# First-layer activation of a two-layer kernel: the square of r moves to ScalarE, and VectorE's two passes become one

## Time and profile before

| what | value |
|---|---|
| median of 3 runs | 1155.81 us (1155.42 to 1156.33) |
| the profiled execution's own time | 1150.71 us |
| span of the profiled execution | 1149.0 us |
| mean granted TensorE clock over the span | 0.993 of full speed |
| busy: TensorE / VectorE / ScalarE | 1125.8 / 947.9 / 630.8 us |
| HBM traffic over the span | 13.70 MB read, 6.29 MB written |

### The profile page before, as it was taken

The page is one execution under the profiler, slowest core; times in us unless marked ns, Lnnn a source line. Parts: engine busy times, 40 slices in busy tenths (PEclk is TensorE's granted clock), DMA queues, the critical chain, the costliest instruction groups (busy, mean ns, idle before and its releaser), DMA issues.

```text
span 1149.0 us, 23218 instructions
## 1 busy us (share of the span) xinstructions
PE 1125.8 (98%) x9746; PEld 951.0 (83%) x9746; DVE 947.9 (83%) x858; ACT 630.8 (55%) x627; POOL 3.4 (0%) x16
## 2 busy tenths in 40 slices
PE   5999999999999999999999999999999999999998
PEld 3777878888888888888888888888888888888886
DVE  7998998978888798888888798887888878866665
ACT  4545655555565655555555555555555555565544
POOL 1000000000000000000000000000000000000000
PEclk8998999999999999999999999999999999999999
DMA  6002300100001000000000000000000000000000
GB/s 183 1 1 65 93 1 1 29 29 1 1 1 29 28 1 1 1 29 28 1 2 1 29 29 1 1 1 29 29 1 2 1 29 1 1 1 1 29 1 28
DMA packets 12423, 21.33 MB, mean 19 GB/s; under 512 B 1073, under 2 KB 5169, under 8 KB 12337
## 3 DMA queue, kind: packets, MB, share of 16 engines
q1 hardware_dynamic: 12256, 19.99, 6.1%
q0 software_dynamic: 64, 0.00, 0.0%
q10 hardware_dynamic: 16, 0.00, 0.0%
HBM read 13.70 MB, written 6.29 MB: 17 GB/s over the span
## 4 chain that ended last, share of the span: by engine, by line
PE 88%; DVE 8%; issue 3%; ACT 1%; DMA 0%; SPq 0%; DVEq 0%; ACTq 0%
PE acc L717 28%; PE h L670 23%; PE h L683 18%; PE acc_rem L732 18%; DVE g L445 3%; DVE g L453 1%; DVE mixed L502 1%; DMA xraw_rem<-in_x 0%; ACT g_hi L303 0%; DVE mixed_rem L516 0%; DVE mixed L516 0%; DVE up_lo L551 0%; DVE up_rem_lo L551 0%; DVE g_lo L463 0%; DVE dn_lo L551 0%
## 5 line engine op out<-in xcount | busy, mean ns | idle before, releaser
L303 ACT ACTIVATE g_hi<-g 128x1024 fp32r<-128x1024 f32 x128 | 135.8, 1061 | 218.8 <-DVE g L453 218.7
L447 DVE SCALAR_TENSOR_TENSOR g<-r,scale,h 128x1024 f32<-128x1024 f32 x128 | 161.9, 1278 | 69.5 <-ACT r L291 69.5
L305 ACT ACTIVATE g_hi<-g,shift 128x1024 fp32r<-128x1024 f32 x128 | 147.6, 1153 | 116.5 <-PE acc_rem L732 101.4
L717 PE MATMUL acc<-g_hi,dn_hi 64*128 64x512 f32 x1024 | 204.7, 389 | 0.4 <-issue 0.4
L732 PE MATMUL acc_rem<-g_lo,dn_rem 64*128 64x512 f32 x1024 | 204.6, 388 | 0.0
L732 PE MATMUL acc_rem<-g_hi,dn_rem 64*128 64x512 f32 x1024 | 204.6, 387 | 0.0
L717 PE MATMUL acc<-g_lo,dn_hi 64*128 64x512 f32 x1024 | 204.3, 388 | 0.0
L717 PE MATMUL acc<-g_hi,dn_lo 64*128 64x512 f32 x1024 | 204.0, 387 | 0.0
L466 DVE SCALAR_TENSOR_TENSOR g_lo<-g,shift,g_hi 128x1024 fp32r<-128x1024 f32 x128 | 164.1, 1282 | 43.6 <-ACT g_hi L305 43.4
L463 DVE TENSOR_TENSOR g_lo<-g,g_hi 128x1024 fp32r<-128x1024 f32 x128 | 156.8, 1225 | 42.9 <-ACT g_hi L303 42.7
L291 ACT ACTIVATE r<-h 128x1024 f32<-128x1024 f32 x128 | 128.1, 1026 | 109.6 <-PE h L683 97.5
(11 more groups left out here) (96 smaller groups left out, 1356.4 us busy)
## 6 DMA issues: line engine op xcount, KB each, us to landing
xraw<-in_x SPq DMA_DIRECT2D x7, 518.0 KB, 4.3
out<-res SPq DMA_DIRECT2D x7, 512.0 KB, 3.3
stage<-in_moe_w_out SPq DMA_DIRECT2D x6, 384.0 KB, 3.4
xraw_rem<-in_x SPq DMA_DIRECT2D x14, 129.5 KB, 4.0
out<-res_rem SPq DMA_DIRECT2D x7, 256.0 KB, 3.6
stage<-in_moe_w_in SPq DMA_DIRECT2D x2, 512.0 KB, 5.4
stage<-in_moe_w_in SPq DMA_DIRECT2D x4, 256.0 KB, 5.1
xraw<-in_x SPq DMA_DIRECT2D x1, 512.0 KB, 4.2
```

What stands on the lines that cost most here:

```text
L303: nc.scalar.activation(g_hi[k][:], g[k][:], ACT.Copy).then_inc(hi_ready, 1)
L305: nc.scalar.activation(g_hi[k][:], g[k][:], ACT.Identity, bias=shift[:, 0:1]).then_inc(hi_ready, 1)
L447: nc.vector.scalar_tensor_tensor(g[k][:], r[k][:], scale[:, 0:1], h[k][:], ALU.mult, ALU.mult).then_inc(h_used, 1)
L717: last = nc.tensor.matmul(acc[:, t, :], w[rows], v[rows, t, :], start=(j == 0 and side == 0 and n == 0), stop=(j == CH - 1 and side == 1 a ...
```

## The change

ScalarE gets one more instruction per first-layer chunk, `square`, which squares r in place and only then gives r_ready. VectorE's `first` becomes one pass that writes the finished g, and `second` is gone. The first layer's `round_g` now waits for h_used as the second layer's does, and `relu` waits for h_used of the chunk two before instead of lo_ready. The order of ScalarE for a first-layer pair becomes relu(a), square(a), relu(b), round_g(a), square(b), then extras, then round_g(b); extras after an even chunk stand between square(a) and relu(b). VectorE's becomes first(a), first(b), low(a), then low(b). TensorE's and the DMA queues' programs are unchanged.

```diff
@@ ScalarE
                 if not (isinstance(S, int) and S < 2):
-                    act.wait_ge(lo_ready, S - 1)
+                    act.wait_ge(h_used, S - 1)
                 if layer == 0:
-                    nc.scalar.activation(r[k][:], h[k][:], ACT.Relu, scale=0.5, bias=half[:, 0:1]).then_inc(r_ready, 1)
+                    nc.scalar.activation(r[k][:], h[k][:], ACT.Relu, scale=0.5, bias=half[:, 0:1]).then_inc(relu_done, 1)
...
-            def round_g(layer, S, k, g_count):
-
-                if layer == 0:
-                    act.wait_ge(g_ready, g_count)
-                else:
-                    act.wait_ge(h_used, S + 1)
+            def square(count, k):
+
+                act.wait_ge(relu_done, count)
+                nc.scalar.activation(r[k][:], r[k][:], ACT.Square).then_inc(r_ready, 1)
+
+            def round_g(layer, S, k):
+
+                act.wait_ge(h_used, S + 1)
...
                     elif j % 2 == 0:
-                        round_g(layer, S0 + j - 1, (j - 1) % 2, G0 + j)
+                        round_g(layer, S0 + j - 1, 1)
                     relu(layer, S0 + j, j % 2)
+                    if j % 2:
+                        round_g(layer, S0 + j - 1, 0)
+                    if layer == 0:
+                        square(G0 + j + 1, j % 2)
                     if j == CH - 1:
                         for f in last or ():
                             f()
-                    if j % 2:
-                        round_g(layer, S0 + j - 1, (j - 1) % 2, G0 + j)
@@ VectorE
                 if layer == 0:
-                    nc.vector.tensor_tensor(g[k][:], h[k][:], r[k][:], ALU.max).then_inc(h_used, 1)
+                    nc.vector.scalar_tensor_tensor(g[k][:], h[k][:], 1.0, r[k][:],
+                                                   ALU.max, ALU.min).then_inc(h_used, 1)
...
-            def second(S, k):
-
-                dve.wait_ge(h_used, S + 1)
-                nc.vector.scalar_tensor_tensor(g[k][:], r[k][:], 1.0, g[k][:],
-                                               ALU.min, ALU.mult).then_inc(g_ready, 1)
...
-                    if layer == 0:
-                        second(S0 + j, j % 2)
```

More of the change, by code:

```diff
@@ L136, in build @@
         h_used = sem("h_used")
-        g_ready = sem("g_ready")
+        relu_done = sem("relu_done")
         hi_ready = sem("hi_ready")
@@ L358, in weights_hi, with phase @@
                     nc.scalar.activation(hi, cols, ACT.Copy).then_inc(w_hi_done, 1)
-            def phase(layer, before, S0, P0, G0, blk_before=None, extras=None, last=None):
+            def phase(layer, before, S0, P0, G0=None, blk_before=None, extras=None, last=None):
                 for j in range(CH):
@@ L366, in phase @@
                         if before is not None:
-                            round_g(before, S0 - 1, 1, G0)
+                            round_g(before, S0 - 1, 1)
                     elif j % 2 == 0:
-                        round_g(layer, S0 + j - 1, (j - 1) % 2, G0 + j)
+                        round_g(layer, S0 + j - 1, 1)
                     relu(layer, S0 + j, j % 2)
+                    if j % 2:
+                        round_g(layer, S0 + j - 1, 0)
+                    if layer == 0:
+                        square(G0 + j + 1, j % 2)
                     if j == CH - 1:
@@ L412, in _ @@
                 S1, P1 = S0 + CH, P0 + 1
-                phase(1, 0, S0, P0, (c + 2) * CH, blk_before=c + 1, extras={
+                phase(1, 0, S0, P0, blk_before=c + 1, extras={
                     6: [lambda: round_mixed_rem(c + 2, X1, S0 - 1)],
@@ L420, in _ @@
             S0, P0 = (LOOPS + 1) * 2 * CH, (LOOPS + 1) * 2
-            phase(1, 0, S0, P0, NB * CH, blk_before=NB - 1, extras={
+            phase(1, 0, S0, P0, blk_before=NB - 1, extras={
                 4: [lambda: round_y(P0 - 1, X1, S0 - 1)],
                 8: [lambda: round_y_rem(NB - 1, X1, S0 - 1)]})
-            phase(1, 1, S0 + CH, P0 + 1, NB * CH, blk_before=NB - 2)
-            round_g(1, S0 + 2 * CH - 1, 1, None)
+            phase(1, 1, S0 + CH, P0 + 1, blk_before=NB - 2)
+            round_g(1, S0 + 2 * CH - 1, 1)
             act.wait_ge(stored, 32 * NB)
```

## The result

| | before | after |
|---|---|---|
| median | 1155.62 us (1154.74 to 1156.33, 4 runs) | 1197.01 us (1194.05 to 1197.45, 4 runs) |
| ratio after to before | | 1.0353, 95% interval 1.0337 to 1.0368 |
| span of the profiled execution | 1149.0 us | 1192.1 us |
| mean granted TensorE clock | 0.993 | 0.992 |

The change makes the kernel 41.4 us, 3.5%, slower. The forecast was 1196.7 us.

A forecast was written before the change was run, and what follows sets the result against it. The prediction took TensorE, busy 98% of the span, as the bound. Loop 35.4, phases 0 and 1 4.4, and first-pair idling 1.1 gave +40.9 us on the median 1155.8: 1196.7 us, range 1182 to 1213.

The forecast's parts named there:

- The chain of a pair: First-layer pair, from relu(a): first(b) ends at 6.78, TensorE goes on at 6.83, 0.44 us after it wants the buffer.
- The period: First-layer pairs of the loop: repeat after 9.18 us instead of 8.63, 0.55 us more per pair.
- One listed sign: TensorE's up_own in first-layer pairs of the loop: idle about 0.3 to 0.44 us on `first` in nearly each.
- The extras: round_y and round_y_rem after even chunks push square(b): 0.58 + 0.92 = 1.5 us more per first-layer phase in the loop.
- Phases 0 and 1: First 16 first-layer pairs, with weight roundings and the first block's end: 154.5 us instead of 150.15, +4.4.
- the first pair: Start of phase 0: TensorE idles during the longer chain and its clock falls, 0 to 2.2 us, taken as 1.1.
- the seam: First block's end, where TensorE waits for the next block's input: kept at 4.7 to 5.3 us over a period.
- The clock: TensorE's granted clock: may fall to 0.50 in phase 0's opening pair, costing 1.1 us; no fall in the loop.
- The sum: Whole kernel: 35.4 us in the loop's six first-layer phases, 4.4 and 1.1 at the start, +40.9 us together.
- The dearer square: Rival, each square on ScalarE: 1.15 us with a bias tile, 11.5 us more, 1208 us in all; chance 0.14.
- the two by which it fits: Rivals, h_used(b) against up_own(b): TensorE never stalls in the loop; 1150 us (chance 0.05) or no difference, 1156 (0.04).
- table loads: Rival, ScalarE: activation table switches for squares, 222 us more, about 1420; chance 0.05, shared with a clock falling in the loop.

The follow-up runs named there:

- three quarters of a square: Changed kernel with each square on 768 of 1024 columns, a quarter of r not squared: 1168.15 us, ratio 1.0117 to the kernel before.
- the order of the squares and the two extras moved: Changed kernel with square(b) ahead of round_g(a), and round_y and round_y_rem after chunks 5 and 9: 1147.60 us, ratio 0.9961 to the kernel before.
- the kernel without `second`: Kernel before with VectorE's second pass left out, g being max(h, r), and round_g released by the first pass: 1142.98 us, ratio 0.9900.
- only the extras moved: Changed kernel with round_y and round_y_rem after chunks 5 and 9, its order of squares kept: 1187.62 us, ratio 1.0300 to the kernel before.
- half a square: Changed kernel with each square on 512 of 1024 columns, half of r not squared: 1155.17 us, ratio 1.0015 to the kernel before.

## Why the prediction was right

Its forecast, 1196.7 us, lies 0.3 us from the median. The mechanism and the terms of the loop came out as written; that the total is so close is partly luck. Between the two profiled executions 40.9 us were forecast and 43.1 measured, and the median of the kernel after lies 1197.01 - 1194.05 = 3.0 us above its profiled execution, where 5.1 was taken over from the kernel before: two errors of 2 us cancel. The steps can be compared one by one.

- **The chain of a pair.** Forecast: round_g(a) 3.50, square(b) 4.46, first(b) 5.56 to 6.78, TensorE at 6.83. Measured: 3.50, 4.47, 5.54 to 6.76, 6.82. The assumed handover inside ScalarE, which no row of before showed, came out at 252.28 - 251.13 - 1.12 = 0.03, as between engines, and the assumed price of the square, 1.06, at 1.053.
- **The period.** Forecast 9.18, measured 9.20: TensorE 0.43 late, 0.11 for the first pass after the stall, the rest in hundredths. One listed sign came out lower: the idle time that the profile gives before up_own(b) is 0.23 in a plain pair, not 0.3 to 0.44, because the pass before it counts as busy for 0.40 of the 0.62 us between the two starts.
- **The extras.** Forecast 0.58 and 0.92 on top. Measured in the kernel after by the starts of relu(a) of the pairs with round_y and round_y_rem: 279.27 - 269.53 = 9.74 and 298.58 - 288.47 = 10.11, that is 0.54 and 0.91.

```profile
269.53 1.12 ACT L289 ACTIVATE r<-h,half 128x1024 f32<-128x1024 f32 x1 [1.34 <-PE h L680]
...
279.27 1.12 ACT L289 ACTIVATE r<-h,half 128x1024 f32<-128x1024 f32 x1 [1.34 <-PE h L680]
...
288.47 1.12 ACT L289 ACTIVATE r<-h,half 128x1024 f32<-128x1024 f32 x1 [1.34 <-PE h L680]
...
298.58 1.12 ACT L289 ACTIVATE r<-h,half 128x1024 f32<-128x1024 f32 x1 [1.34 <-PE h L680]
```

- **Phases 0 and 1.** Forecast 154.5 + 1.1 = 155.6. Measured, by the first relus of the phases in the kernel after (rows that answer to the earlier trace rows, with the second pair of phase 0): 182.14 - 26.15 = 156.0. Of its parts the first pair took 37.22 - 26.15 = 11.07, 1.87 over a normal one where I took 1.1, and the seam 106.47 - 92.86 = 13.61, 4.4 over it where I took about 5.

```profile
26.15 1.12 ACT L289 ACTIVATE r<-h,half 128x1024 f32<-128x1024 f32 x1 [4.64 <-PE h L680]
...
37.22 1.12 ACT L289 ACTIVATE r<-h,half 128x1024 f32<-128x1024 f32 x1 [3.15 <-PE h L680]
...
92.86 1.12 ACT L289 ACTIVATE r<-h,half 128x1024 f32<-128x1024 f32 x1 [1.33 <-PE h L680]
...
106.47 1.12 ACT L289 ACTIVATE r<-h,half 128x1024 f32<-128x1024 f32 x1 [4.89 <-PE h L680]
...
182.14 1.03 ACT L291 ACTIVATE r<-h 128x1024 f32<-128x1024 f32 x1 [1.34 <-PE h L680]
```

- **The clock.** It fell in that first pair, as was held possible, and stayed at 1.00 in the loop (1.00 over 112 to 1130 us). The busy time by stretch, kernel after (length, PE, PEld, DVE, ACT, POOL, clock, DMA share, GB/s):

```profile
27.00:30.00 3.00, 0.51 (x6) 0.20 (x4) 1.23 (x1) 2.60 (x4) 0.00 (x0) 1.00 0.00 0
30.00:36.00 6.00, 5.06 (x24) 3.68 (x25) 4.25 (x6) 3.61 (x5) 0.00 (x0) 0.51 0.00 0
```

TensorE was busy 0.51 of 3 us at the full clock, and then ran at 0.50, the lower level of 1.2 GHz (0.51 is the mean with the start of the second stretch).

- **The sum.** A first-layer phase of the loop was forecast 5.9 us longer. Its pairs measured 9.20 five times, 9.28 at the end, 9.74 and 10.11: a phase took 75.1 us where it took 69.2 before. Six of them make 35.6 us (35.4 forecast) and phases 0 and 1 make 5.8 (5.5 forecast). The first relu came 1.2 later, at 26.15 instead of 24.98, which no term of the forecast holds; it starts anywhere from 24.74 to 26.15 in the profiled executions shown here, and at 25.00 in that of the changed kernel with relu waiting for `low`, so this is not the change's. Together 42.6, where the spans differ by 1192.1 - 1149.0 = 43.1. The medians differ by 41.4.
- **The rivals.** The dearer square did not happen. For the two by which it fits I put the bound at first(b) ending by 6.34; that was too late by up to 0.2 us, as three quarters of a square show. Nor did table loads: the kernel after has one load like the kernel before, and 128 squares of 1.05 us run behind it. That agrees with the Trainium skill, "ScalarE: Activation LUTs", section "Table sets: the hidden batching unit", by which cheap functions are in every set. The list there names relu, copy, identity and abs, not square, so for the square only the trace shows it. The same page's rule in "Rules for kernel authors", to multiply on VectorE, named the better side for this change as it was written, but not for its reason, a faster VectorE: the square took 1.05 us and `second` 1.22, and with the order of the squares and the two extras moved, the form with the square on ScalarE is 0.4% faster than the kernel before.

## What to carry to other kernels

Before work is moved to an idle engine, write out where it lands in that engine's in-order queue, and what the instruction in front of it waits for: here two squares of 1.05 us, on an engine with 45% to spare, cost 0.57 us per pair, because the second stood behind a wait for the very engine that was being relieved. Compare the time at which the last reader of a buffer ends with the time at which the bounding engine wants the buffer back, counted from the weight load of its first pass and not from the pass (here some 0.2 us earlier); below that point added work is free, above it every 0.1 us is paid in every pair. And relief of an engine that is not the bound is worth only what its own late stretches cost, here those of the first 175 us.

## What was not expected of the hardware

A first-layer or second-layer pair in which TensorE never stalls took 8.63 us in most of the loop of the kernel before, and 8.68 in nearly all of the loop of the kernel without `second`, at the same granted clock of 1.00 (138.00 of 138 us busy in both, with 1216 and 1212 matmuls begun):

```profile
300.00:438.00 138.00, 138.00 (x1212) 118.68 (x1210) 98.10 (x87) 75.74 (x74) 0.00 (x0) 1.00 0.04 13
```

Over 128 pairs 0.05 us would be 6 us, which is of the size by which the runs of the kernel before differ among themselves (1150.59 to 1155.51 us on one chip). In the single pairs the difference lies in some ten passes that start 0.23 to 0.24 us apart instead of 0.227. It does not follow the first layer's instructions: second-layer pairs, whose instructions are the same in all of these kernels, took 8.63 in most of the loop of the changed kernel, 8.68 in that with only the extras moved and that with half a square, and now one, now the other in the remaining four. Each kernel has one profiled execution, so whether the pace goes with the kernel or with the execution is not shown. What causes it was not tried and stays open.
